# A chunked recurrence before a feed-forward and an attention layer: solver steps moved to the end of their slot, one copy moved ahead of two others, seven slots of preparation in place of six

## What is computed

```python
# r, k, v, w, a, b: (4, 8, 768, 40)
state = np.zeros((B, H, D, D))
for t in range(S):
    y[:, :, t] = np.einsum('bhd,bhde->bhe', rt, state)
    Sa = np.einsum('bhde,bhe->bhd', state, at)
    state_decay = state * wt[:, :, None, :] - np.einsum('bhd,bhe->bhde', Sa, bt)
    state = state_decay + np.einsum('bhd,bhe->bhde', vt, kt)
# then: ReLU(x @ w_in), a 3-tap convolution over time, a sigmoid gate, @ w_out
# then: four attention experts, the two best per token weighted, @ wo
```

## Time and profile before

| | us |
|---|---|
| median of 3 runs | 1003.91 (1003.06 to 1008.88) |
| the profiled execution: its time | 1005.59 |
| its span | 1003.9 |
| mean granted clock of TensorE | 0.935 of full |
| PE, DVE, ACT, POOL busy | 826.9, 556.5, 312.4, 252.2 |
| first live `g_products` (slot 0) begins | 80.64 |
| tokens for the next layer begin to load | 444.25 |

### The profile page before, as it was taken

One profiled execution on the slowest core, in us unless ns is written; L12 is line 12 of the kernel. 1 busy time (PEld: TensorE's weight loads), 2 busy tenths in 40 slices (PEclk: granted clock), 3 DMA queues, 4 the chain that ended last, 5 costly groups with the idle time before them and its releaser, 6 DMA issues.

```text
span 1003.9 us, 27604 instructions
## 1 busy us (share of the span) xinstructions
PE 826.9 (82%) x11872; PEld 603.9 (60%) x11872; DVE 556.5 (55%) x1235; ACT 312.4 (31%) x739; POOL 252.2 (25%) x524
## 2 busy tenths in 40 slices
PE   2318988897998978859998789997899987899977
PEld 2218888897887978844454555455544545554555
DVE  8686667767776653125436635347355366353464
ACT  3102222223222222212225532235422255312354
POOL 1075856687776876000000000000000000000000
PEclk9999787898777888789999999999999999999999
DMA  3525455565656536232000000100000000000000
GB/s 102 137 57 115 96 131 127 131 147 112 137 121 132 133 73 159 60 101 81 10 31 7 21 14 1 40 1 21 14 7 30 10 12 17 14 1 0 1 21 20
DMA packets 125336, 61.31 MB, mean 61 GB/s; under 512 B 105120, under 2 KB 118048, under 8 KB 123296
## 3 DMA queue, kind: packets, MB, share of 16 engines
q1 hardware_dynamic: 95172, 32.61, 14.5%
q10 hardware_dynamic: 30044, 26.94, 10.4%
HBM read 45.37 MB, written 14.16 MB: 59 GB/s over the span
## 4 chain that ended last, share of the span: by engine, by line
PE 66%; DVE 15%; DMA 7%; ACT 6%; issue 4%; SPq 2%; ACTq 1%; DVEq 0%
PE ps_all L737 9%; PE ps_all L721 8%; PE ps_scan L103 4%; PE ps_all L778 4%; DMA l_by_unit<-l_blocks 3%; PE ps_all L854 3%; PE ps_all L815 3%; PE ps_scan L194 3%; ACT probs L914 3%; PE ps_scan L174 3%; PE ps_all L833 3%; PE ps_all L731 3%; PE ps_all L845 2%; PE ps_all L724 2%; DVE t_update_first L314 2%
## 5 line engine op out<-in xcount | busy, mean ns | idle before, releaser
L314 POOL TENSOR_TENSOR t_update<-l_by_unit,t_by_unit 128x133 f32<-128x133 f32 (+13 forms) x251 | 118.0, 470 | 131.8 <-DVE t_by_unit L316 64.4
L316 POOL TENSOR_TENSOR t_by_unit<-t_by_unit,t_update 128x133 f32<-128x133 f32 (+13 forms) x251 | 128.8, 513 | 19.7
L103 PE MATMUL ps_scan<-decayed_a_and_eye,scaled_then_x 40*128 40x104 f32 x768 | 67.8, 346 | 55.9 <-DVE decayed_a_and_eye L346 55.9
L721 PE MATMUL ps_all<-scaled_then_x,inputs_then_w_up 128*128 128x384 f32 x256 | 91.0, 499 | 15.7 <-DMA scaled_then_x<-y_t 10.0
L103 PEld LDWEIGHTS ps_scan<-decayed_a_and_eye,scaled_then_x 40*128 40x128 f32 x768 | 62.7, 252 | 57.9 <-DVE decayed_a_and_eye L346 42.3
L1005 DVE TENSOR_REDUCE minus_max<-ps_all 128x1 f32<-128x128 f32 (+5 forms) x96 | 54.9, 618 | 75.2 <-PE ps_all L819 75.2
L737 PE MATMUL ps_all<-gated,w_down 128*128 128x384 f32 x256 | 91.1, 499 | 0.0
L721 PEld LDWEIGHTS ps_all<-scaled_then_x,inputs_then_w_up 128*128 128x128 f32 x256 | 48.7, 194 | 52.2 <-issue 12.0
L880 ACT ACTIVATE h<-ps_all 128x384 f32<-128x384 f32 x64 | 28.0, 490 | 148.7 <-PE ps_all L724 148.7
L737 PEld LDWEIGHTS ps_all<-gated,w_down 128*128 128x128 f32 x256 | 46.0, 189 | 44.6 <-issue 19.1
L951 DVE TENSOR_SCALAR conv<-h,w_conv 128x768 f32<-128x768 f32 x32 | 19.9, 621 | 94.7 <-ACT h L880 94.7
(11 more groups left out here) (115 smaller groups left out, 1519.2 us busy)
## 6 DMA issues: line engine op xcount, KB each, us to landing
inputs_then_w_up<-in_x ACTq DMA_DIRECT2D x46, 321.4 KB
r_t_and_v_t<-in_rv ACTq DMA_DIRECT2D x48, 160.0 KB
l_by_unit<-l_blocks SPq DMA_DIRECT2D x24, 256.0 KB, 5.0
uv_and_ruv<-in_v ACTq DMA_DIRECT2D x48, 80.0 KB, 3.0
y_t<-y_out SPq DMA_DIRECT2D x24, 160.0 KB
out<-out_rows SPq DMA_DIRECT2D x24, 160.0 KB, 1.8
l_blocks<-ak_and_l SPq DMA_DIRECT2D x96, 32.0 KB, 2.0
t_blocks<-t_by_unit SPq DMA_DIRECT2D x24, 128.0 KB, 4.7
```

The lines of the kernel that those rows point to most:

```text
L103: last = nc.tensor.matmul(PS[:, o:o + ROWS], weights, AL[c % NK][rows(h), p, :], start=True, stop=True)
L314: return (lambda: eng.tensor_tensor(tmp[:, 0:cols, 0:rest], l[:, s:s + 1, s + 1:BLK].broadcast_to(shape), t[:, 0:cols, s:s + 1].broadcast_ ...
L316: lambda: eng.tensor_tensor(t[:, 0:cols, s + 1:BLK], t[:, 0:cols, s + 1:BLK], tmp[:, 0:cols, 0:rest], ALU.subtract))
L721: nc.tensor.matmul(bank[n][:, 0:HALF], WIN[:, t, cols], XT[:, t, n * HALF:(n + 1) * HALF], start=(t == 0), stop=False)
```

## The change

Five edits in one. GA becomes 7, so the loops begin at slot -7, g_products of slot n belongs to unit n+6 in place of n+5, and the tiles kept per prepared unit become 8 and 9 in place of 7 and 8. `solve_head(j)` goes from the middle of DVE's odd slot 2j-3 (between `suffixes` and `gm`) to the end of the even slot 2j-4. `solve_first` stays behind `gm(3)`, which is now in slot -3. On ACT the copy of corrected x stands ahead of the two copies of B and K. `eye_move` goes from the end of ACT's even slot to behind the y_block copy.

```diff
-GA = 6
+GA = 7
...
             if live: move(YS, PY, "y", "y_sb", n, -1.0)
+            if n % 2 == 0 and 2 <= n // 2 + 2 < NPAIR and n >= 0:
+                eye_move(n // 2 + 2)
             if 2 <= n + GA + 1 < NT: load_x(n + GA + 1)
+            if live: move(ZS, PX, "e", "z_sb", n)
             if ahead: bkn_move(c)
-            if live: move(ZS, PX, "e", "z_sb", n)
             if live: u_move(n)
...
-            if n % 2 == 0 and 2 <= n // 2 + 2 < NPAIR and n >= 0:
-                eye_move(n // 2 + 2)
...
             if prep: suffixes(c)
-            if n % 2 == 1 and 2 <= (n + GA - 3) // 2 < NPAIR: solve_head((n + GA - 3) // 2)
             if ahead: gm(g)
-            if n == -2: solve_first()
+            if n == -3: solve_first()
             if prep: bk(c)
             if 1 <= n and n - 1 < NT - NPAR: state(n - 1)
             if after: y_out(n - 1)
             if prep: al(c)
+            if n % 2 == 0 and 2 <= (n + GA - 3) // 2 < NPAIR: solve_head((n + GA - 3) // 2)
```

## The result

| | before | after |
|---|---|---|
| median of the runs | 1006.39 us (1003.06 to 1011.37, 4 runs) | 1028.29 us (1021.93 to 1037.25, 4 runs) |
| profiled execution, span | 1003.9 us | 1031.1 us |
| PE busy, 11872 matmuls in both | 826.9 us | 856.0 us |
| first live `g_products` | 80.64 us | 91.89 us |
| loading of tokens starts | 444.25 us | 471.54 us |

The change is slower: its time is 1.022 of before's, with a 95% interval of 1.012 to 1.032. In a later comparison the ratio was 1.0229 (1.0152 to 1.0305). The forecast of 996 us and its range up to 1016 both miss it, on the slow side.

A forecast was written before the change was run, and what follows sets the result against it. PE was taken as held up by DVE's solver-step chain and low-clock stretches in odd slots. Slots 4 to 17 -11.0, slots 0 to 3 -2.8, start +7.4, slot 18 -2.0: together -8.4 us, median 996, range 974 to 1016.

The forecast's parts named there:

- The waits that go: Slots 4 to 17: DVE's `l_in` wait falls from 24.6 us to under 5, PE's corrected-x wait from 19.0 to under 3.
- The new wait: In odd slots PE's `g_products` would newly wait for DVE's `hm`, 1 to 3 us.
- third rival: PE idling ahead of `g_products` lowers the whole odd half's clock; pair 32.1 us, total 1015; chance 0.16.
- The even half: Even slots, with the solver steps added on DVE, go from 12.6 to 14.5 us, bounded by DVE.
- The odd half: Odd slots become bounded by PE: 15.2 us at low clock in five pairs, 12.4 at full clock in two.
- The pair: Even plus odd slot, slots 4 to 17: five pairs of 30.2 us and two of 28.6, 208.2 against 219.2.
- The start: An additional preparation round ahead of slot 0 delays `first_blocks(0)` by 7.4 us, about 11 if landings take half as long again.
- Slots 0 to 3: First live slots, mostly PE-bound, have steps in slots 1 and 3; one saved wait gives -2.8 us.
- POOL: Steps overlap POOL's tail, 0.5 us lost per low pair, steps 0.3 to 0.4 us; POOL's wait for DVE under 30.
- ScalarE's order: On ACT, corrected x copied ahead of B and K and `eye_move` behind y: taken as worth 0.

The follow-up runs named there:

- the traffic off: The change with nearly all transfers from unit 4 on cut to one row per block, stores of y whole: 985.15 us, ratio 0.9831.
- The runs with the fill: Extra 128 x 128 matmuls that nothing reads, in each odd live slot; in the change, eight gave ratio 1.0060, sixteen 1.0176.
- the faster start: Seven slots ahead, ACT's new order, steps mid odd slot, first `t_out`/`t_in` ahead of unit 4's `l_out`: 0.9988; with eight extra products 0.9919.
- ScalarE's order alone: Kernel before with only ACT's moves: corrected x ahead of the B and K copies, `eye_move` behind y: 999.29 us, ratio 0.9927.

## Why the prediction was wrong, point by point

- *The waits that go.* Right. `l_in` 0.3 us (forecast under 5), L174 none (under 3).
- *The new wait.* Right in place and size: PE's `g_products` for `hm`, 11.1 us in eight waits in one trace, 4.4 in three in the other, 2.2 us each with the traffic off (forecast 1 to 3). This was the third rival's mechanism.
- *The even half, "14.5 us, bounded by DVE".* This is the first step that failed. The seven even slots took 17.42, 17.13, 17.42, 18.40, 17.27, 17.42 and 16.14 us, 17.3 in the mean. The term "`al` ends 7.1 us in" was read in slot 4 of before, which ran at a clock of 1.00. In slot 4 of after, at 0.70, `al` ends 10.1 us in (152.67 to 162.82), since `g_products` and L194 of PE lie in the chain ahead of it and take 3.74 and 3.00 us for 2.04 and 1.63. The rest was right: steps, `prefixes` and `hm` with the handover came to 7.3 us, 162.82 to 170.09 (forecast 7.4). I had the chain, but priced it as if only DVE's clock mattered.
- *The odd half, 15.2 us low and 12.4 high, two pairs in seven high.* The second. The six odd slots 5 to 15 took 17.64, 17.55, 11.98, 17.36, 18.01 and 17.00; one of six was high, and the low ones were 2.3 us longer than the rows of before at "low". The clock was 0.61 to 0.74 in the low ones, for 0.74 and 0.76 in those rows. The two rows were also no fair sample of a half pair. The even slots just ahead of them, which I did not set beside them, were long:

```profile
240.39:255.20 14.81, 12.54 (x388) 11.87 (x384) 8.95 (x14) 4.49 (x10) 12.75 (x27) 0.93 0.54 126
270.62:286.96 16.34, 14.53 (x387) 13.81 (x384) 9.79 (x18) 4.49 (x10) 13.47 (x29) 0.80 0.66 166
```

So these two pairs took 30.2 and 31.3 us, where the mean pair of before took 31.3, and the forecast joined their short odd halves to an even half of 14.5.

- *The pair.* The forecast's seven pairs were 29.7 us in the mean (208.2 / 7), the measured ones 33.9 (17.3 + 16.6): 4.2 us more, 27 us in the 6.5 pairs of slots 4 to 16. This is the term that decides the result. The third rival had 14.5 + 17.6 = 32.1. Its odd half was right within 0.1 us for the five low slots (17.5 in the mean); it missed the even half, because it let the low clock end where the odd slot ends.
- *The start, +7.4.* Too low: +11.25, the far bound of the estimate, and through the step it named. `g_products` of unit 5 came at 78.99 (forecast 78.1) and `t_out` at 78.81 (78.7), but `t_in` 7.8 us behind it and not 3.6; it is 3.6 again where the transfers beside it are cut.
- *Slots 0 to 3, -2.8.* They gave -6.0, two of them (0 and 1) at a clock of 1.00. The larger gain is luck: no term of the forecast had it.
- *POOL.* Its wait for DVE was to fall under 30 us; it rose to 86.2 from 64.4. With pairs of 34 us the tail of 26.1 and the steps' 4.7 leave POOL idle, and the steps hardly ran beside it: 0.24 us for the one of 78 columns in nine live slots and 0.28 in slot 10, not 0.3 to 0.4. The 0.5 us of overlap per pair was not there.
- *ScalarE's order, 0.* It is worth 0.7% with six slots ahead, where it takes corrected x from behind a late `gm`. With seven ahead no gain of it can be measured (1.0055 without, 1.0079 with). With the steps at the slot's end it is worth 4.6% (1.0686 without, 1.022 with), and the waits of the first point at `eye_move`, whose new place the forecast had only as a cost.
- *The chances.* The third rival got 0.16 with the argument that odd slots are low anyway. The measured loss is beyond its 1015; its mechanism would have been a likelier reading of the trace had the clock been counted on both halves of the pair.

Twice the same error: 0.74 or 0.76 was taken as "the low level's price", where it is a mean of full and half speed that a longer low stretch lowers further. The Trainium skill ("TensorE: Matmul & The Clock Gate", A second HAM failure mode: psum-queue depth-cycling) says of one kernel that short idle spells between groups of matmuls, if frequent enough, make the clock switch back and forth. The runs with the fill agree: with sixteen products in each odd slot the mean clock of slots 0 to 16 went from 0.78 to 0.88.

## What to carry to other kernels

A wait of TensorE has two prices, the idle time and the clock behind it; here idle time of up to some 2 us in front of odd slots, no more than the waits it replaced, came with 15 to 21 us more of busy time than before. So compare busy time for the same count of matmuls before you look for a new wait, and price a chain that passes through TensorE at both levels of its clock. When work is moved out of one engine's critical stretch, look at the very next reader behind its new place: the move can pay only if that reader is late by less than what is taken away, and here even that was not enough. A cheap filler on TensorE shows whether the clock answers, if it is run as well where the gap is not; whether it saves time is read from the stretch and not from the clock. And read a pair of slots that share work as a pair: a short half may have a long one beside it.

## What the runs showed of the hardware that was not expected

- Useless matmuls can pay for themselves: 26.1 us of them in nine slots left the time where it was (1.0010 beside 1.0079), and in the change eight a slot made it 1.6% faster. They do not always: with the faster start the ratio is 0.9919 (0.9850 to 0.9989), but the median of all ten runs, 1002.74 us, is no lower than that of before beside it, 1001.69, so a gain over before is not established. ScalarE's order alone, without a fill, is the one gain that is, 0.9927 (0.9891 to 0.9963).
- PE has gaps that no semaphore explains, about one a slot, of 0.6 to 3.1 us: L201 5.2 us in two, L103 4.4 in three in the list above. They stand at several lines, and where the line is L103 in an odd slot the wait for `hm` is among them. The others shrink with the data traffic: over the recurrence they are 24 and 19 us in the two traces of the change and 9 with nearly all transfers cut, 18 and 11 us in before. How the traffic makes them is open.
- The steps beside POOL and alone: hardly any overlap came about, so the 0.24 and 0.43 us of the earlier trace rows were not tested further.
